# A fused attention, dense layer and expert layer: absolute values and range reduction moved up in their steps, block-diagonal queries for the packed scores, keys turned one step sooner

## The reference

```python
scores = scale * np.matmul(q, k.transpose(0, 1, 3, 2))     # q, k, v: 4 batches, 8 heads, 576 rows, 64 columns
kth = np.partition(scores, -32, axis=-1)[..., -32:-31]
scores = np.where(scores >= kth, scores, -1e9)
attn = softmax(scores)
x = attn @ v                                               # reshaped to 2304 tokens x 512

h = x @ w_in                                               # 512 -> 2048
x = (h * np.cos(h)) @ w_out                                # 2048 -> 512

e_idx = argmax(x @ w_gate)                                 # 8 experts, 512 -> 1024 -> 512
out[mask] = gate_w * eom * (relu(x[mask] @ w1[e]) @ w2[e])
```

## Time and profile before

| | us |
|---|---|
| median of three runs (1356.54 to 1361.6) | 1360.67 |
| the profiled execution | 1360.97 |
| its span, first to last instruction | 1358.9 |
| PE busy | 1245.0 (92%) |
| DVE busy | 851.5 (63%) |
| ACT busy | 641.1 (47%) |
| POOL busy | 554.2 (41%) |

### The profile page before, as it was taken

One profiled execution on the slowest core, in us unless ns is written; L12 is line 12 of the kernel. 1 busy time (PEld: TensorE's weight loads), 2 busy tenths in 40 slices (PEclk: granted clock), 3 DMA queues, 4 the chain that ended last, 5 costly groups with the idle time before them and its releaser, 6 DMA issues. The chain is left out here.

```text
span 1358.9 us, 18020 instructions
## 1 busy us (share of the span) xinstructions
PE 1245.0 (92%) x5962; PEld 792.3 (58%) x5963; DVE 851.5 (63%) x1690; ACT 641.1 (47%) x1082; POOL 554.2 (41%) x624
## 2 busy tenths in 40 slices
PE   4568999999999999999999999897599999999996
PEld 2446756857658668477577576584244444444443
DVE  6999996998998998988879989042211111111110
ACT  3555765775776766856757757340011111111110
POOL 2544662564754654735636636324211211112110
PEclk9667999999999999999999999898699999999998
DMA  7301001101001100100100000012414443251000
GB/s 239 115 9 26 9 26 26 34 9 34 9 25 35 26 24 1 26 25 18 44 24 1 8 9 1 16 68 73 144 33 155 158 149 143 74 190 70 15 14 1
DMA packets 81836, 71.49 MB, mean 53 GB/s; under 512 B 62266, under 2 KB 62266, under 8 KB 81248
## 3 DMA queue, kind: packets, MB, share of 16 engines
q1 hardware_dynamic: 76192, 60.86, 14.0%
q0 software_dynamic: 5568, 9.65, 2.2%
HBM read 62.97 MB, written 11.45 MB: 55 GB/s over the span
## 5 line engine op out<-in xcount | busy, mean ns | idle before, releaser
L728 DVE MAX8 tops<-scores_left 128x8 f32<-128x576 f32 x432 | 307.8, 762 | 0.0
L994 PE MATMUL dense_banks<-weights,h_T 128*128 128x512 f32 x512 | 235.5, 603 | 16.3 <-POOL h_T L434 16.3
L414 POOL TENSOR_TENSOR probs<-scores,probs 128x576 f32<-128x576 f32 x144 | 212.1, 1495 | 69.8 <-ACT probs L525 69.7
L983 PE MATMUL dense_banks<-x_T,weights 128*128 128x256 f32 x1024 | 234.9, 382 | 0.0
L730 DVE MATCH_REPLACE8 scores_left<-tops,scores_left 128x576 f32<-128x576 f32 x288 | 213.7, 757 | 0.0
L983 PEld LDWEIGHTS dense_banks<-x_T,weights 128*128 128x128 f32 x1024 | 189.4, 190 | 36.2 <-issue 13.1
L1136 PE MATMUL dense_banks<-weights,expert_h_T 128*128 x400 | 183.8, 592 | 0.0
L1117 PE MATMUL score_banks<-weights,x_gathered_T 128*128 x400 | 182.7, 600 | 1.0 <-DVE x_gathered_T L871 1.0
L994 PEld LDWEIGHTS dense_banks<-weights,h_T 128*128 128x128 f32 x512 | 93.0, 192 | 121.9 <-issue 95.8
L728 DVE MAX8 tops<-scores 128x8 f32<-128x576 f32 x144 | 102.4, 757 | 79.8 <-ACT scores L539 79.7
L424 POOL TENSOR_SCALAR probs<-probs,reciprocals 128x576 f32<-128x576 f32 x144 | 133.5, 938 | 6.0 <-DVE reciprocals L735 5.9
(11 more groups left out here) (160 smaller groups left out, 1592.0 us busy)
## 6 DMA issues: line engine op xcount, KB each, us to landing
weights<-in_moe_w SPq DMA_DIRECT2D x16, 2048.0 KB, 10.9
y_rows<-y_rows_sb SPq DMA_DIRECT2D x18, 256.0 KB, 2.0
k_rows<-in_k SPq DMA_DIRECT2D x32, 128.0 KB, 2.6
q_rows<-in_q SPq DMA_DIRECT2D x16, 256.0 KB, 3.4
v_rows<-in_v SPq DMA_DIRECT2D x32, 128.0 KB, 2.3
weights<-in_moe_w_in SPq DMA_DIRECT2D x1, 4096.0 KB, 13.0
weights<-in_moe_w_out SPq DMA_DIRECT2D x1, 4096.0 KB, 23.2
k_rows<-in_k SPq DMA_DIRECT2D x16, 32.0 KB, 2.5
```

Of the source, the lines that this page charges most:

```text
L414: nc.gpsimd.tensor_tensor(ex, SS[:, u % 3, i, :], ex, ALU.subtract).then_inc(s["masked_done"], 1)
L728: V.max(top, src).then_inc(s["tops_done"], 1)
L983: last = MM(HO[:, f % 2, 0:BT], win[:, kd, f * P:(f + 1) * P], XT[:, m % 2, kd, :], start=kd == 0, stop=kd == KD - 1)
L994: last = MM(HO[:, t, :], HS[:, f, t * P:(t + 1) * P], wout[:, f, :], start=f == 0, stop=f == NF - 1)
```

## The change

Four edits. First, in `keys_turned` and in SP's loads of keys 2 and 3, `FINAL + 1 == s` becomes `FINAL == s`. Second, DVE's folding: at i = 2, part 0 stands ahead of the turn's first `max` and part 1 behind the first pair; at i = 4 both stand one pair sooner. Third, ACT's absolute values: the two instructions go ahead of `copy_x`; at i = 2 one stands on each side of the last `copy_h`. Fourth, a tile q_T_blocks holds the queries of a packed tile with zeros off the diagonal blocks; POOL zeroes it once, ACT fills it with two copies of 64 rows in place of one of 128, and PE makes the packed scores with one product over the whole array where two stood.

```diff
@@ -80,7 +80,7 @@
 
     out = [(0, s + 1)] if s + 1 < HP else []
     for b in range(1, B):
-        out += [(b, p) for p in range(HP) if FINAL[b - 1, p] + 1 == s]
+        out += [(b, p) for p in range(HP) if FINAL[b - 1, p] == s]
     return out
 
 
...
+        QB = sb("q_T_blocks", [P, 2, HP, P], stack=att)
...
@@ -342,7 +344,7 @@
                         store_rows(2 * m + 1)
                 for b in range(1, B):
                     for p in range(2, HP):
-                        if FINAL[b - 1, p - 2] + 1 == st:
+                        if FINAL[b - 1, p - 2] == st:
                             load_keys(b, p)
 
             sp.wait_ge(s["late_filled"], len(LATE_BANK))
@@ -399,6 +401,10 @@
             const(pool.memset(table_init[:, :, 1], 0))
             const(pool.iota(table_init[:, :, 0], [[0, ROWS // P]], base=NOBODY, channel_multiplier=0))
             pool.wait_ge(s["const_ready"], n_const[0])
+            pool.memset(QB[0:D, :, :, D:2 * D], 0.0).then_inc(s["blocks_zeroed"], 1)
+            pool.wait_ge(s["blocks_zeroed"], 1)
+            pool.memset(QB[D:2 * D, :, :, 0:D], 0.0).then_inc(s["blocks_zeroed"], 1)
+            pool.wait_ge(s["blocks_zeroed"], 2)
             pool.dma_start(table.rearrange("(p s) w -> p s w", p=P), table_init[:]).then_inc(s["table_written"], 16)
 
             def consts(u):
@@ -576,7 +582,12 @@
                      small(("k", b, p, 1))[:, 0:REM].unsqueeze(1).to_broadcast([P, 2, REM])).then_inc(s["small_emptied"], 1)
 
             def copy_queries(t):
-                copy(QT[:, t % 2, :, :].rearrange("p a n -> p (a n)"), small(("q", t))).then_inc(s["small_emptied"], 1)
+                if t % 9 == 4:
+                    two = small(("q", t)).rearrange("p (a b n) -> p b a n", a=HP, b=2)
+                    copy(QB[0:D, :, :, 0:D], two[0:D, :, :, :])
+                    copy(QB[D:2 * D, :, :, D:2 * D], two[D:2 * D, :, :, :]).then_inc(s["small_emptied"], 1)
+                else:
+                    copy(QT[:, t % 2, :, :].rearrange("p a n -> p (a n)"), small(("q", t))).then_inc(s["small_emptied"], 1)
 
             def copy_yT(t):
                 copy(YT[:, :, :].rearrange("p a n -> p (a n)"), small(("t", t))).then_inc(s["small_emptied"], 1)
@@ -584,11 +595,10 @@
             def copy_logits(t):
                 copy(L[:, t, :], small(("g", t))[:, 0:2 * E]).then_inc(s["small_emptied"], 1)
 
-            def absolute(m, g):
+            def absolute(m, g, h):
                 act.wait_ge(s["reduced_done"], m * 4 + 2 * g + 2)
-                for h in range(2):
-                    r = R[:, g, h * 4:h * 4 + 4, :]
-                    nc.scalar.activation(r, r, ACT.Abs).then_inc(s["cos_done"], 1)
+                r = R[:, g, h * 4:h * 4 + 4, :]
+                nc.scalar.activation(r, r, ACT.Abs).then_inc(s["cos_done"], 1)
 
             def sine(m, g, h):
                 act.wait_ge(s["cos_done"], m * 8 + 4 * g + h + 1)
@@ -642,7 +652,12 @@
                             sine(m, (i - 3) // 2, h)
                     if i < 4:
                         copy_h(m, 4 * i + 2)
+                    if i in (2, 4):
+                        absolute(m, (i - 2) // 2, 0)
+                    if i < 4:
                         copy_h(m, 4 * i + 3)
+                    if i in (2, 4):
+                        absolute(m, (i - 2) // 2, 1)
                     if i in (6, 7):
                         copy_y(2 * m + i - 6)
                 if 0 <= u < NS:
@@ -659,9 +674,6 @@
                     copy_queries(queries_turned(st))
                 for b, p in keys_turned(st):
                     copy_keys(b, p)
-                for m, i in dense:
-                    if i in (2, 4):
-                        absolute(m, (i - 2) // 2)
                 if st >= LOOP - 2:
                     late_copy(LAST[0], st - (LOOP - 2))
 
@@ -747,15 +759,20 @@
                                            op0=ALU.mult, op1=ALU.add).then_inc(s["reduced_done"], 1)
 
             for st in range(LOOP):
+                for m, j in block_at(st):
+                    if j == 2:
+                        reduce_h(m, 0, 0)
                 for op in range(7):
                     for i in range(2):
                         if st < NS:
                             top_op(st, i, op)
                         if op == 2 and i == 1 and 0 <= st - 2 < NS:
                             reciprocals(st - 2)
-                    for m, i in block_at(st):
-                        if i in (2, 4) and op in (1, 2):
-                            reduce_h(m, (i - 2) // 2, op - 1)
+                    for m, j in block_at(st):
+                        if j == 2 and op == 0:
+                            reduce_h(m, 0, 1)
+                        if j == 4 and op < 2:
+                            reduce_h(m, 1, op)
 
             chain = [0]
 
@@ -920,12 +937,11 @@
                 at_least(pe, s["scores_copied"], st)
                 at_least(pe, s["probsT_copied"], st - LAG)
                 if sp_.packed:
+                    pe.wait_ge(s["blocks_zeroed"], 2)
                     for x in range(2):
                         for g in range(2):
-                            for h in range(2):
-                                a = slice(h * D, (h + 1) * D)
-                                last = MM(SPB[a, 2 * x + g, 0:HALF], QT[a, qa, sp_.p + x, sp_.c0:sp_.c0 + 64],
-                                          KT[a, sp_.p + x, REM + g * HALF:REM + (g + 1) * HALF], start=True, stop=True)
+                            last = MM(SPB[:, 2 * x + g, 0:HALF], QB[:, sp_.c0 // 64, sp_.p + x, :],
+                                      KT[:, sp_.p + x, REM + g * HALF:REM + (g + 1) * HALF], start=True, stop=True)
                 else:
                     for g in range(2):
                         for h in range(2):
```

More of the change, by code:

```diff
@@ L250, in build @@
                  "table_written rows_ready ids_cleared experts_loaded xgT_filled xgT_copied "
-                 "eh_done relu_done ehT_done ehT_copied slot_done y_scaled tri_done oh_ready "
+                 "eh_done relu_done ehT_done ehT_copied slot_done y_scaled blocks_zeroed tri_done oh_ready "
                  "pe_waits pool_waits").split()
```

## The result

The changed kernel takes 1341.58 us (median of four runs, 1341.33 to 1343.67), the kernel before 1361.09 beside it (1356.54 to 1361.60). The ratio is 0.987, with a 95% interval of 0.984 to 0.989. The forecast was 1345, with 1337 to 1353. The profiled execution took 1343.67, with a span of 1342.1; before these were 1360.97 and 1358.9. Beside the later runs the kernel before took 1356.56, 1359.23 and 1356.90, so across them ratios are compared, and not times.

What follows compares the result with a forecast made beforehand. PE was taken as the bound (busy 690.57 of 712.44 us), DVE close behind. Terms 5.1 + 2.1 + 0.1 + 4.1 + 1.7 + 0.7 + 1.7 = 15.5 off 1360.97 gave 1345.5, forecast 1345 us, range 1337 to 1353.

Steps and rivals of the forecast that it cites:

- the end: Behind the last scores: DVE starts its last turn 2.4 us sooner relative to PE, needs 0.7 more; 1.7 us gained.
- the folding at i=2: Turn 45: part 0 fits DVE's idle time, part 1 misses POOL's mask; PE's 1.02 wait goes in five blocks, 5.1 us.
- The folding at i=4: Turns 47 and 48: PE's 0.64 wait for turned probabilities vanishes in three blocks, 2.1 us; wait for product and second block, 0.1.
- Rival B: At i=4 part 1 gets ahead of POOL's mask, turn 47 takes 13.1 us; time 1338, chance 0.20.
- The absolute values: On ACT at i=2 and i=4: they cover ACT's wait for h; gain already in DVE's chain, not counted again.
- The keys: Keys turned one turn sooner: waits of 0.64 for key copies go; turns 16 to 18, 32 to 36, 52 to 54, 4.1 us.
- Rival C: Key turns give nothing: turn 16's wait behind the sines equals what goes, clock falls there; 1351 to 1353, chance 0.18.
- The clock: Turn 19's scores: with the waits of turn 18 gone, the lower clock behind them goes; 1.7 us.
- The packed scores: Eight whole-array passes take 2.1 us where sixteen on quarters take 2.16; 8 x 0.09 = 0.7 us gained.
- A: The forecast itself, with its own range by the terms of 1341 to 1350; chance 0.50.
- D: ACT takes up DVE's earlier end, so POOL's products come when they did; only keys and clock remain, 1356, chance 0.08.
- E: Slower: packed scores draw full passes (11 us) or new waits hold the clock down (13.6 a slice); 1370, chance 0.04.

Runs made afterwards that it cites:

- the better kernel: The changed kernel with the folding at i=4 back behind the second and third pair: 1332.54 us, ratio 0.982; run again, 1334.11 us, ratio 0.982.

## Why the prediction held, and where its steps failed

The time (1341.6 for 1345) came out right, and that is in part luck. Within M I forecast 13.8 (15.5 less the end's 1.7) and it was 16.7; at the end I forecast 1.7 and it was 0.2. By edits the terms are further off than by turns: the folding at i=2 was priced at 5.1 and gave 16.6 alone, the one at i=4 was priced at a gain of 2.2 and costs 5.6 once the other is made. The two errors cancel for the most part.

**The folding at i=2: right in mechanism, its size too small.** The wait at i=4 is gone in five blocks: 5.3 for 5.1. Part 1 takes 2.27 as forecast. But I stopped there, and gave what follows in turns i=5 and i=6 to the other edit. The run with this edit alone shows it has all of i=5 too (3.6) and 2.9 at i=6.

**The folding at i=4: the step that failed.** I priced i=5 at 0.64 + 0.07 a block; the turn fell by 1.21, and the folding at i=2 alone gives all of it. In turn 48 the 10.95 us that I took for PE's work were 0.49 more than the 10.46 of the changed kernel. No row labels this as waiting; a part lies ahead of the first turned probabilities, which came 4.94 after the scores (561.22, just as ACT's copy of scores ended at 561.17) and now come 4.71 after them. PE therefore reached turn 49 that much sooner, and the wait at i=6 stayed 1.51 where I had 1.24. The length of turn 47 was sized well (14.4, measured 14.12; part 1 3.4, measured 3.13), as was the second block (1.3, measured 1.44 with turn 25 at 11.97). What I did not ask is what the edit would be worth **once the other was made**: I compared with the kernel before, where turn 47 took 14.1 anyway, and not with a kernel with the folding at i=2 alone, where it takes 13.18. That was the larger question: 5.6 us. Rival B saw the right object, POOL's small instruction held by part 0, and asked it only for the chance that part 1 gets ahead.

**The absolute values.** "Not counted again" nearly held inside the change (0.5 gained) and was wrong by itself (7.0 lost, 3.6 of it clock). The reason given, that they cover ACT's wait for h, needs part 1 to be done by then: in the changed kernel ACT has no wait for it in turn 53, with the move alone it has 3.25.

**The keys: 4.1 forecast.** Turns 16 to 18 gained 2.1 (1.5), turns 32 to 36 1.0 (0.5), turns 52 to 54 3.0 (2.1). But the folding at i=2 alone has 2.9 of that. The clean figure is the kernel with the folding at i=4 and the absolute values both back against the one with the folding at i=2 alone, 695.8 - 690.1 = 5.7 of M for keys and packed scores together, or 4.8 for the keys after the 0.9 of the packed scores: a little over the forecast. The wait for x in turn 16 came as forecast (1.2):

```profile
186.70 0.27 PE L924 MATMUL small_banks<-ident,k_rows 64*128 64x64 f32 x1 [1.26 <-ACT x_T L565]
```

Rival C (nothing from the key turns) is what the keys alone show in turns 16 to 36; it failed in the whole because the earlier DVE lifts what is waited for there.

**The clock: 1.7 forecast, 1.7 measured** in turn 19 (15.76 to 14.08 with the folding at i=2 alone; 13.83 with the packed scores as well). It needs no key: each of the two foldings alone kept the clock up at 217 too, and the keys alone only moved the fall to 188. The start of that turn, for the last of the earlier trace rows, at full clock:

```profile
213.69:217.00 3.31, 3.31 (x17) 2.74 (x16) 0.98 (x3) 1.95 (x4) 0.20 (x1) 1.00 0.03 6
```

**The packed scores: right, but for the 0.09.** 2.1 us and 0.7 in all were forecast; 2.11 to 2.21 for a row and 0.9 were measured. The rate by columns, 0.25 for a pass of 288, was the right end of the bounds. The 0.09 a turn does not follow from the terms beside it, which give 2.0 + 0.16 = 2.16, as much as before; it comes out only by the time to the next product, 2.09 less 2.00, where 0.05 to 0.15 were measured. The Trainium skill (TensorEngine Tiling (Array Packing), Theoretical Speedup) gives dimensions up to 64 a speedup of up to 2x when tiled. The trace agrees: a whole-array pass cost about two quarter passes (0.25 for 0.13).

**The end: right, and then given back.** From the last scores to the products behind the last wait it took 25.77 before (857.61 - 831.84) and 23.94 now, 1.8 for the 1.7 forecast:

```profile
839.18 6.64 PE L1010 MATMUL dense_banks<-weights,h_T 128*128 128x512 f32 x8 [2.35 <-POOL h_T L440]
```

But these products took 6.64 for the 5.90 of the earlier trace rows, since the clock was low for more of them, and from their end to the span's end it took 496.3 for 495.4 before. So all behind M gained only 0.2 us. One execution each can't settle a difference of that size: in the better kernel, run twice, the time behind turn 71 was 519.6 and 523.4.

Of the rivals, A's range held the time. B did not come in turn 47, where part 1 took 3.13; that a few hundredths of a microsecond can decide who is first, the two executions of the better kernel show in turn 71. D and E are out: the waits went, and the clock stayed full through M.

## What to carry to other kernels

Price each of several moves on top of the others, not on the kernel before: here one was worth +5.7 alone and -5.6 in company, another -7.0 alone and +0.5 in company. Where two engines exclude each other by whole instructions, place a long one by where the other's instruction boundaries fall then, and count the small instructions that it holds up ahead of them, since these set the boundaries. A wait that is moved ahead of a copy is only as good as the producer is early.

## What the runs showed of the hardware

- DVE's two folding instructions and POOL's instructions kept each other out for whole instructions. Part 1 takes 2.27 when POOL runs nothing at its start; begun under a POOL instruction it took 2.15 and that one's remainder (2.41 with 0.26 left, 3.10 with 0.95, 3.13 with 0.98, 3.47 with 1.32). POOL's small products of 0.20 or 0.21 us took 1.08 to 1.20 under part 0, or 0.72 where part 0 was half over, and 2.10 under part 1 (the changed kernel's POOL, turn 45):

```profile
518.55 2.10 POOL L425 TENSOR_SCALAR denominators<-sums 128x2 f32<-128x2 f32 x1 [2.10 <-ACT probs L539]
```

MAX8 and MATCH_REPLACE8 held nobody up: in M of all traces each took 0.73 to 0.80, beside POOL's mask or not, and half a mask took its 1.41 beside them. I had used the standing still, but had not expected that an instruction on 128x2 elements, held, could be what saves the next one.
- Which of the two engines is first can differ between executions of one kernel: part 1 in turn 71, begun 0.07 and 0.09 us behind POOL's second half of the mask by the record, took 2.29 in one and 3.47 in the other.
- The last wait of 2.34 or 2.35 us is in all fourteen traces. In thirteen the clock fell behind it (5.16 to 6.64 us for products that take 3.70), in one it stayed full. That one is the execution with the shortest wait ahead of it, 0.41 us for the turned probabilities; the others had 0.70 to 1.69. That the shorter wait is the reason is not shown. A single run's tail is no ground for a verdict of 4 us here.
- Not settled: whether a place for the folding at i=4 exists in which the wait at i=6 goes altogether in turns 41, 49 and 65, as it did in turn 25 with part 0 ahead of the turn. The sum above speaks against it.
